# Moving the split of the first expert matrix to the end of a turn in a routed two-layer kernel

## The reference, cut to what matters

```python
logits = x @ w_gate                       # x: 3072 tokens x 320
expert_idx = np.argmax(logits, axis=1)
...
for e in range(8):
    xe = x[expert_idx == e]
    h = np.maximum(xe @ w1[e], 0.0)       # w1[e]: 320 x 1024
    out[mask] = gate_w[mask, None] * (h @ w2[e])   # w2[e]: 1024 x 320
```

## Time and profile before

| what | value |
|---|---|
| median of 3 runs | 823.92 us (820.87 to 824.55) |
| the profiled execution | 820.93 us, span 819.0 us |
| granted TensorE clock, mean | 0.991 |
| TensorE busy | 763.2 us, 93% of the span |
| VectorE, ScalarE, GpSimd busy | 72%, 52%, 39% |
| HBM read, written | 105.63 MB, 9.33 MB |

### The profile page before, as it was taken

One profiled execution on the slowest core, in us unless ns is written; L12 is line 12 of the kernel. 1 busy time (PEld: TensorE's weight loads), 2 busy tenths in 40 slices (PEclk: granted clock), 3 DMA queues, 4 the chain that ended last, 5 costly groups with the idle time before them and its releaser, 6 DMA issues. The chain is left out here.

```text
span 819.0 us, 17200 instructions
## 1 busy us (share of the span) xinstructions
PE 763.2 (93%) x5765; PEld 741.7 (91%) x5765; DVE 593.1 (72%) x1006; ACT 423.7 (52%) x649; POOL 319.0 (39%) x297
## 2 busy tenths in 40 slices
PE   2788999999999999999999999979859999999994
PEld 1788999999999999999999999979859999999994
DVE  4653868787878787878878788568667676867850
ACT  3023445454545454545454555655466676767751
POOL 2442544534343445454444544540633323232111
PEclk9999999999999999999999999999988999999998
DMA  6962222222222223232333200542987535545300
GB/s 202 313 168 75 77 92 76 91 75 91 75 91 75 92 81 93 81 96 87 94 86 98 86 24 1 177 123 65 297 303 243 186 108 193 165 153 169 114 21 5
DMA packets 41457, 97.05 MB, mean 119 GB/s; under 512 B 6935, under 2 KB 24481, under 8 KB 39754
## 3 DMA queue, kind: packets, MB, share of 16 engines
q1 hardware_dynamic: 37498, 87.46, 33.7%
q0 software_dynamic: 3920, 9.08, 4.1%
HBM read 105.63 MB, written 9.33 MB: 140 GB/s over the span
## 5 line engine op out<-in xcount | busy, mean ns | idle before, releaser
L545 POOL TENSOR_TENSOR g_t<-u_t,r_t 128x512 f32<-128x512 f32 x96 | 135.8, 1415 | 255.5 <-ACT u_t L695 255.4
L690 ACT ACTIVATE r_t<-bank,neg 128x512 f32<-128x512 f32 x96 | 66.0, 687 | 186.8 <-PE bank L1384 186.8
L1396 PE MATMUL bank<-wo_h,g_h 128*128 128x328 f32 x384 | 127.3, 332 | 2.1 <-DVE g_l L1006 2.1
L1000 DVE TENSOR_SCALAR u_t<-bank 128x512 f32<-128x512 f32 x96 | 66.0, 688 | 75.6 <-ACT r_t L690 52.0
L1396 PE MATMUL bank<-wo_h,g_l 128*128 128x328 f32 x384 | 120.1, 313 | 0.0
L1396 PE MATMUL bank<-wo_l,g_h 128*128 128x328 f32 x384 | 120.1, 313 | 0.0
L627 POOL DMA_INDIRECT out_x<-ob,idx_tok x31 | 38.2, 1234 | 155.0 <-ACT ob L765 150.7
L695 ACT ACTIVATE u_t<-u_t,half 128x512 f32<-128x512 f32 x96 | 69.4, 723 | 40.9 <-DVE u_t L1000 39.7
L936 DVE TENSOR_TENSOR_SCAN W<-W,cst 128x512 f32<-128x512 f32 x48 | 83.4, 1740 | 4.9 <-DMA W<-decays 4.9
L1517 PE MATMUL bank<-w_h,h_h 128*128 128x320 f32 x248 | 78.4, 316 | 2.6 <-DVE w_l L1061 1.5
L1384 PE MATMUL bank<-xT_h,wi_h 128*128 (+1 forms) x384 | 78.8, 287 | 1.6 <-issue 1.6
(11 more groups left out here) (231 smaller groups left out, 1953.3 us busy)
## 6 DMA issues: line engine op xcount, KB each, us to landing
raw<-in_w SPq DMA_DIRECT2D x12, 1280.0 KB
W<-decays SPq DMA_DIRECT2D x24, 512.0 KB, 5.1
raw<-in_w SPq DMA_DIRECT2D x12, 1024.0 KB
raw2n<-in_w SPq DMA_DIRECT2D x7, 1280.0 KB
raw1n<-in_w SPq DMA_DIRECT2D x7, 1024.0 KB
raw<-in_w SPq DMA_DIRECT2D x24, 256.0 KB
qG<-in_q SPq DMA_DIRECT2D x24, 180.0 KB
qT<-in_qt SPq DMA_DIRECT2D x48, 80.0 KB
```

Of the source, the lines that this page charges most:

```text
L545: pool.tensor_tensor(g_t[p % 2][:, :], u_t[p % 2][:, :], r_t[p % 2][:, :], ALU.add).then_inc(sm["g_done"], 1)
L690: act.activation(r_t[p % 2][:, :], bank_h[p % 2][:, :], ACT.Relu, bias=neg1[:, 0:1]).then_inc(sm["r_done"], 1)
L1000: dve.tensor_scalar(u_t[p % 2][:, :], bank_h[p % 2][:, :], 1.0, -1.0, ALU.min, ALU.max).then_inc(sm["u_done"], 1)
L1396: mm = pe.matmul(bank_acc[tt][:, 0:DL], l[p % 4][:, c], r[:, f, :], start=f == 0 and a == 0, stop=f == NT1 - 1 and a == 2)
```

## The change

The two calls of `w1_high(s + 2, .)` on ScalarE and of `w1_low(s + 2, .)` on VectorE leave their place at the start of turn s. In a turn whose next slot is wide, half 0 now stands between `h_high(s + 1, 2)` and `h_high(s + 1, 3)`, and half 1 behind `h_high(s + 1, 3)`; where the next slot is narrow, both stand behind the split of its second matrix. The same on VectorE. TensorE's, SP's and GpSimd's lists stay as they are, and so do the instructions.

```diff
@@ ScalarE, loop over s
                     h_plain(s, 1)
                 if s + 1 < NS:
                     y_high(s + 1)
-                if s + 2 < NS:
-                    w1_high(s + 2, 0)
-                    w1_high(s + 2, 1)
                 if s >= 1:
                     out_gate(s - 1)
                 if KINDS[s] == "H":
@@
                         h_high(s + 1, 1)
                         w2_high(s + 1, 1)
                         h_high(s + 1, 2)
+                        if s + 2 < NS:
+                            w1_high(s + 2, 0)
                         h_high(s + 1, 3)
+                        if s + 2 < NS:
+                            w1_high(s + 2, 1)
                     else:
                         w2_high(s + 1, 0)
                         w2_high(s + 1, 1)
+                        if s + 2 < NS:
+                            w1_high(s + 2, 0)
+                            w1_high(s + 2, 1)
@@ VectorE, loop over s
                 if s + 1 < NS:
                     y_low(s + 1)
-                if s + 2 < NS:
-                    w1_low(s + 2, 0)
-                    w1_low(s + 2, 1)
                 if KINDS[s] == "H":
                     hT_low(s, 0)
                     hT_low(s, 1)
@@
                         h_low(s + 1, 2)
+                        if s + 2 < NS:
+                            w1_low(s + 2, 0)
                         h_low(s + 1, 3)
+                        if s + 2 < NS:
+                            w1_low(s + 2, 1)
                     else:
                         w2_low(s + 1, 0)
                         w2_low(s + 1, 1)
+                        if s + 2 < NS:
+                            w1_low(s + 2, 0)
+                            w1_low(s + 2, 1)
```

## The result

| | before | after |
|---|---|---|
| median, us | 823.26 (4 runs) | 847.5 (4 runs, 846.77 to 848.48) |
| ratio, 95% interval | | 1.0294 (1.0271 to 1.0316) |
| profiled execution, span | 819.0 | 845.3 |
| granted clock, mean | 0.991 | 0.979 |

The change costs 24.2 us by the medians. The forecast was 843 us, range 834 to 851, with a chance of 0.88 for slower. The spans of the two profiled executions differ by 26.3 us, of which 1.49 us lie ahead of anything that the change touches.

A forecast was written before the change was run, and what follows sets the result against it. TensorE, busy 93% of the span, was taken as the bound. Terms for turn 3 (-1.4) and slots 5, 8, 11, 14, 16, 18 total 20.8 us on 820.93: 841.7, or 844.7 by the median; forecast 843, range 834 to 851.

The forecast's parts named there:

- turn 3: Old stall passes to slot 4's second matrix, landing at 611.5; 8.56 us shrinks to about 7, gain 1.8 us.
- SP's order as the decisive step: In SP's list the second-matrix reload stands behind a first-matrix reload awaiting the moved split; issued 3.4 us after it.
- two signs of being wrong: Prediction wrong if L729 does not wait for a DMA after 620 us, or the stall at 606 is gone.
- A: Rival, faster: the old stall in turn 3 simply goes, giving 815 us; chance 0.07.
- B: Rival, no change: reloads of slots 5 and 11 come in time after all, 823.6 us; chance 0.05.
- C: Rival, slower by less: slot 11's load nearly in time, or clock stays up and slot 5's at lower bound; 834; chance 0.12.
- D: Rival, slower by more: late first matrices meet their users, or indirect transfers lengthen pairs to 13 us; 852 and over; 0.06.
- Slot 5: ScalarE waits 8.15 us for slot 5's late second matrix, plus 2.1 of clock; wait bounds 6.9 to 10.3.
- Slot 11: ScalarE waits 5.2 us for slot 11's second matrix, plus 2.1 of clock, besides a small stall of 0.87.
- The clock: Long idle time of TensorE is followed by half clock, costing 2.1 us each for slots 5 and 11.
- The small stalls: Behind narrow slots TensorE waits for `y_low`: 0.87 us at slots 8, 11, about 0.8 at 14, 16, 18, some 0.4 at 5.
- Slot 8's late signal: At slot 8 both reloads are skipped, yet the late signal costs 0.2 to 2 us; 0.5 taken.

The follow-up runs named there:

- e1: Changed kernel with SP's loop asking for the second matrix before the first matrix: 825.69 us, ratio 1.0035.
- e2: Kernel before with the split moved in turn 3 alone: 833.64 us, ratio 1.0136.
- e3: Changed kernel with slot 8's second matrix really loaded where it is otherwise skipped: 855.6 us, ratio 1.0402.
- e4: Changed kernel with extra unused TensorE products, 76 in slot 5 and 54 in slot 11, during the long waits: 841.63 us, ratio 1.0229.
- e8: Changed kernel with the two gathers for slot 15 moved behind the scatter of slot 10: 843.7 us, ratio 1.0272.
- e13: e1 with the second half of the first matrix's split moved behind the next turn's split of the tokens: 820.7 us, ratio 0.9975.
- e5: Changed kernel with the loop order of e1, and slot 4's second matrix asked for before slot 5's first ahead of the loop: 822.65 us, ratio 1.0008.
- e6: Kernel before, split at its old place, with the same two SP orders as e5: 835.72 us, ratio 1.0173.
- e10: e7 with slot 6's first matrix loaded behind slot 5's first ahead of the loop: 821.58 us, ratio 0.9978.
- e11: Kernel before with only the loads ahead of the loop reordered as in e10: 825.84 us, ratio 1.0018.
- e12: Kernel before, split moved in turn 3 alone (second half as e7), e10's loads ahead of the loop, slot 5's second before slot 7's first: 820.77 us, 0.9948.
- e7: e5 with the second half of the first matrix's split moved behind the next turn's split of the tokens: 815.57 us, ratio 0.9928.

## Why the prediction came out as it did

**What bounds the kernel, and turn 3: right.** The old wait at L721 went and L729 took it over, 6.59 us long. Slot 4 starts 1.49 us later than before, so times of turns 3 and 4 are compared less 1.49: the load is there at 613.05 - 1.49 = 611.56 (611.5 in the sum). The six other kernels with the split moved in turn 3 and the loads ahead of the loop in the old order (e1 to e4, e8, e13) have 611.2 to 611.6, taken in the same way, so the match is not chance. TensorE's stall of 8.56 became 6.84 and the gain up to slot 5 was 1.23 us. e5 shows the cause: with that load earlier the wait at L729 is gone.

**SP's order as the decisive step: right**, shown by e1 (0.0259 of 0.0294 come back), e2 (one turn's move makes slot 5's loss) and e3 (slot 8 escapes only by its skipped load). Neither of the two signs of being wrong came: L729 waits twice behind 620 us, and TensorE still stands 6.84 us in turn 3. The rivals A, B and C fell. Of D, slot 11's first matrix, with its margin of 1.6 us, did not make ScalarE wait; indirect transfers did lengthen the loads, but slot 5's pair took 11.77 us and not 13.

**The terms that were mis-sized** are the two long waits. Slot 5: from the first matrix's issue to the landing of the second I took 9.8 + 0.5 us and got 637.39 - 625.62 = 11.77, which is inside the bound of 12; the wait grew with it, 9.39 for 8.15. Slot 11: 4.7 + 0.3 reckoned, 6.85 measured, 6.83 us of wait for 5.2. e8 names the main part: I put two gathers and a scatter at 0.3 us where the gathers alone cost 1.45. The 4.7 had also been read to the last byte and not to the start of the instruction that waits: with the gathers gone, e8 moves its last bytes before 725 us, 4.8 us after the issue, and L731 starts after 5.40. For slot 5 the same two causes are likely, but no run tries them; the stretches of the changed kernel show its last bytes between 636 and 637 us, ahead of L729 at 637.39.

**The clock: right in kind, short for slot 11.** TensorE's idle time before the fourth unit is usually 0.29 us, so 9.64 and 7.08 are 9.35 and 6.79 more than usual. The growth less that is 11.57 - 9.35 = 2.2 us for slot 5 (2.1 forecast) and 9.59 - 6.79 = 2.8 for slot 11 (2.1 forecast). e4 got back 5.3 for the two by the medians, 4.5 by the traces.

**The small stalls: right in place**, 0.9 us each, also where I had reckoned 0.8; e13 gives them back at their forecast worth. Before slot 5 it was 0.15 for some 0.4. Slot 8's late signal cost 0.23 for 0.5.

**The sum and the range.** The errors of the terms add up to 3.9 us, nearly all on one side, so the closeness is not owed to errors that cancel. The range was less well founded than it looks. The bounds given for turn 3, slot 5 and slot 8 add up to about -3 and +5 us, not -5 and +7; slot 11, where the forecast missed most (9.59 for 7.3), was given no bounds at all. The rest was margin, and it wasn't needed.

The wrong numbers of the experiments teach more. In e5, e6 and e10 to e12 I reckoned what one load gains and not what it takes from its neighbours: in the kernel before the transfer share is 0.97 from 580 to 600 us and 0.91 or more in each microsecond from 602 to 612 (the earlier trace rows show 440 GB/s in one of these).

## What to carry to other kernels

A step that reads a buffer is also the step that sets it free: moving it late moves the reload and, in a list that is worked in order as SP's is here, every reload listed behind. Write the order of the loads down beside the order of the steps that free their buffers and change both together; here the first-first order went with the early split and the second-first order with the late one, and the wrong pairing cost some 1.4% one way and 2.9% the other. Move a step only in the turns where something waits behind it: here that was turn 3 alone. Where an engine waits first for one load, look for the next load in line before counting on the gain.

## What the runs showed of the hardware that was not expected

Two indirect gathers of 164 KB each, beside a load of 1.31 MB, delayed its use by 1.45 us, more than their 0.33 MB at the 369 to 399 GB/s of the load's full stretches in e8 (0.8 to 0.9 us, an estimate). The start of slot 4 lies between 602.16 and 606.65 us in eight profiled executions whose instructions up to there are the same (before, after, e1 to e4, e8, e13): a spread of 4.5 us whose cause is open, which is why the stretches above are compared from that point on. An idle time of 2.52 us left the clock at 2.4 GHz (e7); one of 3.45 (e10, granted clock 0.50 from 630 to 633 us) and one of 3.77 (e5) were followed by 1.2 GHz.
